# A two-stage fp32 MLP kernel on Trainium2: VectorE's part of the first weight split in two pieces, another bank order in the last solo steps, two GpSimd splits by halves

## What is computed

```python
w = softmax(weight)                                   # 8 heads x 7 taps
x = einsum('hk,bskhg->bshg', w, windows(x))           # 2 x 4096 tokens, 192 wide
h = x @ moe_w_in                                      # 192 -> 2048
g = where(h >= 1, h, where(h <= -1, 0, (h + 1)**2/4)) # first MLP's gate
x = g @ moe_w_out                                     # 2048 -> 192
h = x @ moe2_w_in
out = (h * sigmoid(1.702 * h)) @ moe2_w_out
```

## Time and profile before

| | us |
|---|---|
| three runs | 1142.23, 1141.12, 1142.29; median 1142.23 |
| the profiled execution | 1142.78 |
| its span, first to last instruction | 1141.0 |
| TensorE busy | 1128.8 (99%) |
| VectorE busy | 826.2 (72%) |
| ScalarE busy | 704.3 (62%) |
| GpSimd busy | 465.9 (41%) |
| TensorE's granted clock, mean | 0.998 |

### The profile page before, as it was taken

The page is one execution under the profiler, slowest core; times in us unless marked ns, Lnnn a source line. Parts: engine busy times, 40 slices in busy tenths (PEclk is TensorE's granted clock), DMA queues, the critical chain, the costliest instruction groups (busy, mean ns, idle before and its releaser), DMA issues.

```text
span 1141.0 us, 25656 instructions
## 1 busy us (share of the span) xinstructions
PE 1128.8 (99%) x9384; PEld 1023.6 (90%) x9384; DVE 826.2 (72%) x1180; ACT 704.3 (62%) x1227; POOL 465.9 (41%) x455
## 2 busy tenths in 40 slices
PE   8999999999999999999999999999999999999998
PEld 5878988999999999999999999999999998899887
DVE  7888777777777777777777777777777777766633
ACT  5886666656566565666656656566666556665554
POOL 6997754180723617145180632707236180000000
PEclk9999999999999999999999999999999999999999
DMA  6312112020010200102011020200202000000000
GB/s 178 100 44 70 40 22 52 2 53 12 16 49 2 56 8 15 49 8 54 4 41 24 12 53 1 55 10 15 50 5 55 6 16 16 11 6 1 15 6 24
DMA packets 108950, 35.84 MB, mean 31 GB/s; under 512 B 101042, under 2 KB 105394, under 8 KB 108848
## 3 DMA queue, kind: packets, MB, share of 16 engines
q1 hardware_dynamic: 108848, 34.34, 12.7%
HBM read 22.50 MB, written 6.29 MB: 25 GB/s over the span
## 4 chain that ended last, share of the span: by engine, by line
PE 92%; POOL 3%; DVE 2%; ACT 1%; SPq 1%; DMA 1%; issue 0%; DVEq 0%; POOLq 0%; ACTq 0%
PE h_all L842 4%; PE h_all L847 4%; PE h_all L845 4%; PE h_all L819 4%; PE h_all L849 4%; PE h_all L851 4%; PE acc_all L921 4%; PE acc_all L924 4%; PE acc_all L913 4%; PE acc_all L918 4%; PE acc_all L916 4%; PE h_all L821 4%; PE acc_all L886 4%; PE acc_all L888 4%; PE h_all L832 4%; PE h_all L829 4%
## 5 line engine op out<-in xcount | busy, mean ns | idle before, releaser
L1118 ACT ACTIVATE g_hi<-h_all 128x512 fp32r<-128x512 f32 x256 | 153.6, 600 | 223.5 <-PE h_all L853 196.4
L1282 DVE TENSOR_TENSOR g_lo<-gate,g_hi 128x512 fp32r<-128x512 f32 x232 | 196.0, 845 | 104.0 <-ACT g_hi L1108 98.0
L1287 DVE TENSOR_TENSOR g_lo<-h_all,g_hi 128x512 fp32r<-128x512 f32 x256 | 177.0, 691 | 121.7 <-ACT h_all L1121 120.2
L1108 ACT ACTIVATE g_hi<-gate 128x512 fp32r<-128x512 f32 x232 | 146.4, 631 | 140.7 <-DVE gate L1276 139.0
L1267 DVE TENSOR_SCALAR clip<-h_all 128x512 f32<-128x512 f32 x256 | 175.9, 687 | 42.6 <-PE h_all L851 40.1
L595 POOL TENSOR_TENSOR x_conv<-x_conv,prod 128x384 f32<-128x384 f32 (+1 forms) x174 | 190.4, 1094 | 2.5
L1102 ACT ACTIVATE clip<-clip,half 128x512 f32<-128x512 f32 x256 | 182.8, 714 | 9.2 <-DVE clip L1267 8.6
L589 POOL TENSOR_TENSOR prod<-x_in,tap_w 128x384 f32<-128x384 f32 (+1 forms) x174 | 167.9, 973 | 7.5
L1276 DVE TENSOR_TENSOR gate<-h_all,clip 128x512 f32<-128x512 f32 x232 | 160.5, 692 | 7.1 <-ACT clip L1102 1.7
L589 POOL TENSOR_TENSOR x_conv<-x_in,tap_w 128x384 f32<-128x384 f32 (+1 forms) x29 | 31.9, 1102 | 297.4 <-DVE x_rest_a L1335 150.3
L1121 ACT ACTIVATE h_all<-h_all 128x512 f32<-128x512 f32 x256 | 152.3, 595 | 0.0
(11 more groups left out here) (289 smaller groups left out, 4699.9 us busy)
## 6 DMA issues: line engine op xcount, KB each, us to landing
x_in<-in_x SPq DMA_DIRECT2D x14, 960.0 KB, 4.9
out_y<-raw SPq DMA_DIRECT2D x360, 16.0 KB, 1.4
raw<-x_conv SPq DMA_DIRECT2D x336, 16.0 KB, 1.8
raw<-in_moe_w_out SPq DMA_DIRECT2D x6, 384.0 KB, 3.9
raw<-in_moe_w_in SPq DMA_DIRECT2D x8, 256.0 KB, 3.9
raw<-in_moe_w_in SPq DMA_DIRECT2D x3, 512.0 KB, 3.1
x_in<-in_x SPq DMA_DIRECT2D x2, 384.0 KB, 5.4
stage<-in_moe_w_out SPq DMA_DIRECT2D x2, 384.0 KB, 5.6
```

Of the source, the lines that this page charges most:

```text
L1108: nc.scalar.activation(g1_hi[step.s % G_RING][:, :], gate1_of(step)[:, :], ACT.Copy).then_inc(g1_hi_ready, 1)
L1118: nc.scalar.activation(gate2_hi(step)[:, :], src, ACT.Gelu_apprx_sigmoid).then_inc(g2_hi_ready, 1)
L1282: nc.vector.tensor_tensor(g1_lo[k][:, :], gate1_of(step)[:, :], g1_hi[k][:, :].bitcast(FP32), ALU.subtract).then_inc(g1_lo_ready, 1)
L1287: nc.vector.tensor_tensor(gate2_lo(step)[:, :], bank2(step)[:, :], gate2_hi(step)[:, :].bitcast(FP32), ALU.subtract).then_inc(g2_lo_ready, 1)
```

## The change

1. `LO_CUTS` has four pieces of 256 columns. GpSimd still does the first two. VectorE's subtraction of 512 columns in front of its first slot is gone; in slot 0 behind the clip of step 0, and in slot 1 behind the clip of step 1, it does one piece of 256 columns each. Step 4 waits for the first of them, step 6 and the load of chunk 6 for both.
2. In slot 2 TensorE runs two matmuls on a zeroed operand (`warm_up`, fp32, 256 columns) into a free bank, between the up matmuls of step 3 and the down matmuls of step 0.
3. Solo steps 16 to 23 take the banks in the order 0, 2, 1, 3. Waits are worked out from the bank's last user: step 17 now waits for the residue of step 14 (was 13), step 18 for that of 13 (was 14); in `begin_up` step 24 waits for that of 20 as before, the second MLP's step 0 for that of 21 (was 22), step 25 for that of 22 (was 21), the second MLP's step 1 for that of 23 as before.
4. GpSimd subtracts chunks 12 and 13 in two halves of 512 columns each, with one semaphore increment after the second.

```diff
@@ -254,8 +254,16 @@
         def alone1(step):
             return isinstance(step.n, int) and step.n < BEHIND
 
+        def solo_bank(n):
+
+            return n % SOLO_BANKS if n < F_TILES else (0, 2, 1, 3)[n % SOLO_BANKS]
+
+        def last_in_bank(bank, n):
+
+            return max(k for k in range(min(n, BEHIND)) if solo_bank(k) == bank)
+
         def bank1(step):
-            return h[step.n % SOLO_BANKS] if alone1(step) else h[step.s % 2]
+            return h[solo_bank(step.n)] if alone1(step) else h[step.s % 2]
 
         def gate1_of(step):
 
@@ -365,7 +373,7 @@
 
         FIRST_CUTS = [slice(0, 4 * P), slice(4 * P, IN_CHUNK)]
 
-        LO_CUTS = [slice(0, 2 * P), slice(2 * P, 4 * P), slice(4 * P, IN_CHUNK)]
+        LO_CUTS = [slice(k * 2 * P, (k + 1) * 2 * P) for k in range(4)]
 
         def raw_before(n):
             if n in STAGED:
@@ -426,8 +434,8 @@
                 kind, c = CHUNKS[n % N_CHUNKS]
                 before = raw_before(n)
                 if before == 0:
-                    sp.wait_ge(w_ready, len(LO_CUTS) - 1)
-                    sp.wait_ge(w_last_ready, 1)
+                    sp.wait_ge(w_ready, 2)
+                    sp.wait_ge(w_last_ready, 2)
                 elif before == 1:
                     sp.wait_ge(rest0_ready, W_PIECES)
                 elif before is not None:
@@ -631,7 +639,14 @@
                     nc.gpsimd.tensor_tensor(lo[0], raw_view(n)[:, :, 0:DM], hi[:, :, 0:DM].bitcast(FP32),
                                             ALU.subtract).then_inc(wp_ready, 1)
                 else:
-                    nc.gpsimd.tensor_tensor(lo, raw_view(n), hi.bitcast(FP32), ALU.subtract).then_inc(wp_ready, 1)
+
+                    pieces = 2 if n > 2 * N_CHUNKS - 5 else 1
+                    size = IN_CHUNK // pieces
+                    for k in range(pieces):
+                        cols = slice(k * size, (k + 1) * size)
+                        ins = nc.gpsimd.tensor_tensor(lo[:, cols], raw_view(n)[:, cols], hi[:, cols].bitcast(FP32),
+                                                      ALU.subtract)
+                    ins.then_inc(wp_ready, 1)
 
 
             for k in range(1, ACT_TAPS_0):
@@ -777,13 +792,15 @@
                     if step.s == 4:
                         pe.wait_ge(w_last_ready, 1)
                         pe.wait_ge(rest0_ready, W_PIECES)
+                    if step.s == 6:
+                        pe.wait_ge(w_last_ready, 2)
                     if step.s == F_TILES // 2:
                         pe.wait_ge(wp_ready, chunk_of(0, "rest", 1) + 1 - FIRST_CHUNKS)
                 if step.s == 0:
                     pe.wait_ge(x_from_dve, (step.tile + 1) * 2)
 
                 if step.n >= SOLO_BANKS:
-                    pe.wait_ge(g1_lo_ready, step.n - SOLO_BANKS + 1)
+                    pe.wait_ge(g1_lo_ready, last_in_bank(solo_bank(step.n), step.n) + 1)
                 five(bank1(step)[:, :], 0, step.s, x_set[step.side]).then_inc(h1_ready, 1)
 
             def up2(step):
@@ -804,7 +821,7 @@
                     pe.wait_ge(x_from_dve, (one.tile + 1) * 2)
                 if isinstance(one.n, int) and one.n < BEHIND + 2:
 
-                    pe.wait_ge(g1_lo_ready, one.n - SOLO_BANKS + 1)
+                    pe.wait_ge(g1_lo_ready, last_in_bank(one.s % 2, BEHIND) + 1)
                 else:
                     pe.wait_ge(gate1_ready, one.n - 1)
                 nc.tensor.matmul(bank_1, in_hi[0][LOWER, cols1], x_hi[LOWER, :], start=True, stop=False)
@@ -813,7 +830,7 @@
                 if two.s == 0:
                     pe.wait_ge(y_from_dve, (two.tile + 1) * 2)
                 if isinstance(two.n, int) and two.n < 2:
-                    pe.wait_ge(g1_lo_ready, BEHIND - 1 + two.n)
+                    pe.wait_ge(g1_lo_ready, last_in_bank(2 + two.s % 2, BEHIND) + 1)
                 else:
                     pe.wait_ge(g2_lo_ready, two.n - 1)
                 nc.tensor.matmul(bank_2, in_hi[1][UPPER, cols2], y_hi[UPPER, :], start=True, stop=False)
@@ -1028,6 +1045,10 @@
                     up1(back(tile, side, s, -1))
                 if n == FIRST_PREP_STEP:
                     transpose_x(1, acc1)
+                if n == SOLO_LAG:
+
+                    for _ in range(2):
+                        warm_up(acc1[0], HALF_TT)
                 if n >= SOLO_LAG and n != FIRST_PREP_STEP + 1:
                     down1(back(tile, side, s, SOLO_LAG))
                 if n == FIRST_PREP_STEP:
@@ -1344,6 +1365,12 @@
                 nc.vector.tensor_tensor(rest[0:DR, :], banks[1][DR:P, :], rest[DR:P, :].bitcast(FP32),
                                         ALU.subtract).then_inc(x_from_dve, 1)
 
+            def split_in(part):
+                dve.wait_ge(w_hi_ready, 3)
+                hi, lo = (v[:, LO_CUTS[part]] for v in split_views(0))
+                nc.vector.tensor_tensor(lo, raw_view(0)[:, LO_CUTS[part]], hi.bitcast(FP32), ALU.subtract
+                                        ).then_inc(w_last_ready, 1)
+
             def prepare_x(tile, side, s):
                 at = prep(tile)
                 for part in at["turn"].get(s, ()):
@@ -1373,6 +1400,8 @@
                     residue1(before1)
                 if one is not None:
                     clipped(one)
+                if isinstance(tile, int) and tile == 0 and s < 2:
+                    split_in(2 + s)
                 if solo and before1 is not None:
                     residue1(before1)
                 if takes_y(tile) and solo and at_y == 4:
@@ -1456,9 +1485,6 @@
             dve.wait_ge(x_from_act, 2)
             nc.vector.tensor_tensor(x_rest[0:DR, :], x_rest_sum, x_rest[DR:P, :].bitcast(FP32), ALU.subtract
                                     ).then_inc(x_from_dve, 1)
-            dve.wait_ge(w_hi_ready, 3)
-            hi, lo = (v[:, LO_CUTS[-1]] for v in split_views(0))
-            nc.vector.tensor_tensor(lo, raw_view(0)[:, LO_CUTS[-1]], hi.bitcast(FP32), ALU.subtract).then_inc(w_last_ready, 1)
             run_head(slot)
             with nc.Fori(0, LOOP_PAIRS, engines=(dve.engine,), hint_back_edge=True) as i:
                 run_body(slot, i)
```

## The result

The changed kernel takes 1139.26 us (median of 13 runs, 1138.85 to 1139.88) where the kernel before takes 1141.94 (13 runs, 1141.12 to 1142.88). The ratio is 0.9977 with a 95% interval of 0.9968 to 0.9985: 2.7 us faster, 1.7 to 3.7. The forecast was 1139.0 with a range of 1137.7 to 1140.7, and a chance of 0.70 for faster, which it let begin at 1139.95; so time and sign came out as said. Whether the reasons did is the subject of the rest, and for one of the four terms they didn't.

The account below looks back on a forecast made before the run. TensorE is 99% busy, so only its stalls and slow stretches can pay. Head 0.95, banks 1.63 - 0.1 and halves 0.75 sum to 3.2 us, taking the median from 1142.23 to 1139.0 (range 1137.7 to 1140.7).

Parts of the forecast that it names:

- clock term: Around the first down matmuls: with TensorE's long gap broken up, the granted clock stays up and 1.34 us comes back.
- the head: Kernel start, up to the first down matmuls: split pieces and warm-ups together gain 1.4 us (0.8 to 2.1).
- Part 1: Kernel start: VectorE's split in two pieces moves the stall behind the third down matmul; alone 0.05 us (-0.55 to +0.75).
- Place B: First tile's end, near 51 us: GpSimd's end limits TensorE's transposes, so 0.95 us (0.72 to 1.1) of 1.4 comes through.
- Part 3: Step 24, near 74 us: new bank order lets the second MLP's step 0 start earlier; 1.63 us kept, less 0.1.
- The rival that the weight load waited for w_down and not for the bank: Step 24: second MLP's step 0 waits for GpSimd's w_down, so some 0.6 us instead of 1.63; chance 0.06.
- Part 4: Near 90 us: halved GpSimd splits hold VectorE's residue at most 1.84 us, TensorE doesn't wait; 0.75 us (0.5 to 0.85).
- Place E: Near 149 us, where VectorE waits 2.54 us for moved blocks of x: stall stays as it is, 0.
- "slower" rival: Near 149 us: GpSimd doesn't move with TensorE, VectorE's wait grows to 4.8 us, clock falls; 1142.7 us, chance 0.04.

Follow-up runs that it names:

- e9: Kernel before with GpSimd's last addition for tile 1 left out; 1141.10 us, ratio 0.9990.
- e2: Kernel before with only the new bank order 0, 2, 1, 3 in steps 16 to 23; 1141.13 us, ratio 0.9989.
- e12: e11 with the old head: VectorE's split in one piece of 512 ahead of clip 0, no warm-up matmuls; 1138.43 us, ratio 0.9970.
- e3: Kernel before with only GpSimd's subtractions of chunks 12 and 13 cut in halves; 1141.12 us, ratio 0.9995.
- e6: Kernel before with only the two warm-up matmuls added; 1142.06 us, ratio 1.0002.
- e1: Kernel before with only VectorE's split in two pieces behind the clips and the two warm-up matmuls; 1141.94 us, ratio 0.9999.
- e10: e1 with GpSimd's last addition for tile 1 left out; 1141.36 us, ratio 0.9992.
- e11: Changed kernel with tile 3's moves of x issued in two halves, the first after GpSimd's first four heads; 1137.90 us, ratio 0.9962.
- e4: Changed kernel with GpSimd's subtractions of chunks 12 and 13 undivided again; 1140.38 us, ratio 0.9985.
- e5: Changed kernel without the two warm-up matmuls; 1139.87 us, ratio 0.9983.

## Why the prediction came out, step by step

**The clock term was the wrong one (1.34 of the head's 1.4).** Its arithmetic was right for the one execution that was profiled; the error was to take it for what the kernel always does. Six traces have VectorE's split ahead of the first clip: before (gap 1.83, fall), e9 (1.80), e2 (1.69), e12 (1.60), e3 (1.52) and e6 (0.69, with warm-ups), and only the first has the fall. What it costs when it comes is confirmed: from the fourth down matmul to the second down step pass 2.98 in before and 24.96 - 23.35 = 1.61 in e9. A fall shows in a run's mean granted clock as well. By the windows of before it takes away 1.7 us of full clock, 0.0015 of the run, so a run with a fall is at 0.9985 or less. Of the 98 runs of before beside the experiments 53 are listed at 1.000 and can't have one; 7 are at 0.998 as the profiled execution is. The 38 at 0.999 stay open, since after has that mean too with its clock at 1.00 up to the last matmul. So at most 45 of the 98 have a fall, at the head or at step 24. The 7 have a median of 1142.59, the 53 one of 1142.12: by this a fall costs the whole time some 0.5. The median of the three runs of before, 0.55 below its profiled execution, had said as much, and the prediction used the difference only to shift its result.

**The gap that goes was nearly worthless without the clock.** Part 1 by itself was put at 0.05 (-0.55 to +0.75), and this was the right size for the whole head. The measure is the time from the start of step 0's last up matmul to the second down step, which leaves out when the input arrived: 8.16 in before with its fall, 6.37 to 6.60 in the five other old heads, and 6.38 to 6.70 in the five new heads whose first piece won the race (6.38 in after), 7.23 to 7.49 in the three where it lost. The first down matmul does come 0.6 to 0.9 earlier, then TensorE waits for the residue; the prediction had said that "the stall moves behind the third down matmul" and had put the fourth at 23.1 instead of 23.16, so that the second down step stays where it was.

**Place B caps, as said, and more firmly.** The rule that GpSimd's end of tile 1 takes all but 0.95 was right in kind. Only, TensorE waits 0.81 to 1.11 for it in the old kernel too whenever the clock stays up (e12, e6, e3, e2). In the old head without a fall, TensorE's arrival leaves nothing to gain at place B, so of 0.95 there remains what the falls cost in the executions that have one. The medians put the head at 0.2 (e1 against before), -0.3 (e10 against e9), 0.5 (e11 against e12) and 0.7 (e4 against e2), each with an uncertainty of about 1. Their average is 0.3, and anything between 0 and 0.7 fits; e1 alone can't settle it.

**Part 3 was right.** 1.63 less 0.1 was forecast; 1.61 in after and 1.56 in e2 were measured. The rival that the weight load waited for w_down and not for the bank is refuted by the traces of e2 and after: with the bank free both partners start at once. The transfer to the next stall, which the prediction covered by part 4, shows in e2 and e4.

**Part 4 was right in mechanism and, as far as medians tell, somewhat small.** Forecast 0.75; the medians say 1.0 alone and 0.9 to 1.1 in place, each with an uncertainty of about 1. In place the stall to be prevented is the one of 0.83 in chunk 13, which the prediction had named as the danger and not priced as a gain. The residues took 1.12, 1.36 and 1.75 against the limit of 1.84.

**Place E was right**: 0. The shift of 3.47 passes through it whole; GpSimd moved with TensorE at slot 30, so the "slower" rival lacked its condition. The idle time of GpSimd fell by 2.48, from 6.02 to 3.54, and was not used up.

**The sum.** Forecast 0.95 + 1.53 + 0.75 = 3.2; measured 2.7. By the average above the head fell short by some 0.7, and the halves brought 0.2 to 0.3 more; none of these differences is clear of the noise by itself. The parts measured alone add up to 0.2 + 1.0 + 1.0 = 2.2. The profiled pair differs by 3.9, since it holds the clock fall, and GpSimd's early end of 0.28. The predicted median of 1139.0 was near 1139.26 partly by luck: errors of opposite sign cancel among the terms, and the median of before, from which 3.2 was taken, came out 0.3 lower in 13 runs (1141.94) than in the three (1142.23).

**Of what should be seen**: clip 0 at 18.30 (18.4), first down matmul 21.26 (21.5), fourth 22.53 (23.1) behind a wait for the residue of 0.34 (0.8), clock 1.00, the wait ahead of the transposes 0.85 (0.5). The stall ahead of the fourth is smaller because VectorE came to the second piece at 20.99 and not at 21.3, and met a GpSimd operation that ended at 21.60 and not at 22.1. The Trainium skill, "VectorE: DVE Perf Modes", section on the TRN2 errata, gives by its formula, as an estimate, 0.42 for 256 columns. No run here can confirm it: the piece that won took 0.43, but each of the pieces in the eight traces met a GpSimd operation, and its length is set by that.

**Still open**: what decides whether the clock falls behind a gap of 1.1 to 1.8; how often it does; how often the first piece loses its race; the 0.6 between e5 and after, where e5's trace has a stall of 1.17 at place E instead of 0.80; the head's exact worth, and the 0.5 between e11 and e12 in particular.

## What to carry to other kernels

Ask of every loss in a profiled execution whether the median has it too: where the profiled time lies above the median, look for an event such as a clock fall, and don't put its full price on the change that removes it. An engine that comes earlier gains only up to the next one that it waits for, so look for the wait that would appear if the stall were absent, here GpSimd's end of the tile. Cut the GpSimd operations that a neighbour on the critical path can meet; and where an order hangs on less than 0.1 us between two engines, count both outcomes.

## What the hardware showed that was not expected

- Idle time of TensorE doesn't decide alone whether the granted clock falls: 1.15 us were followed by 0.50 (e6, step 24) where 1.14 to 1.16 were not (before, e1, e3, e9 and e10, same place), and 1.52, 1.60, 1.69 and 1.80 were not at the head where 1.83 were.
- VectorE's subtraction of 256 columns takes 0.43 to 0.75 when it comes late in a GpSimd operation of 256 columns, 0.89 in the middle of one of 480 columns, and 1.54 to 1.58 at the very start of one of 512. In all 16 cases of the eight traces its end lies 0.27 to 0.32 behind that of GpSimd's operation; none met no operation. The other way round, GpSimd's 512 columns take 1.46 to 1.51 instead of 1.29.
- SyncE needs about 0.7 us for each move of 16 KB (24 in 16.55, 12 in 8.69), so a row of them can be later than the engine that waits for them.
